# Token mixing as two f32r passes per tile, and an earlier load of layer one's second weights

## What is computed

```python
attn_out = _attn_ref(q, k, v, s)                 # 4 batches, 8 heads, 576 tokens, 64 wide; causal softmax with a bias
x = attn_out.transpose(0, 2, 1, 3).reshape(4, 576, 512)
# first layer
xn = (x - mu) / np.sqrt(var + 1e-06) * g_ln
x = x + np.maximum(xn @ w_ch1, 0.0) @ w_ch2       # 512 -> 2048 -> 512
# second layer, with token mixing
h = x.transpose(0, 2, 1) @ U @ V                  # U is 576x32, V is 32x576
u = x + h.transpose(0, 2, 1)
out = u + np.maximum(u @ w_ch1, 0.0) @ w_ch2
```

## Time and profile before

| | |
|---|---|
| median of 3 runs | 1120.89 us (1119.97 to 1123.44) |
| the profiled execution, time and span | 1120.59 us, 1118.7 us |
| busy, whole span | PE 1056.2, DVE 802.1, ACT 545.7, POOL 338.2 us |
| PE on the chain that ended last | 91% |
| attention | 0 to about 280 us |
| layer one, layer two | to about 725 us, to the end |
| mean clock granted to PE | 0.992 |

### The profile page before, as it was taken

How to read it: one execution, slowest core, us unless ns; L and a number is a source line. 1 busy time by engine, 2 the same in 40 slices (tenths; PEclk the granted TensorE clock), 3 DMA queues, 4 the chain that set the end, 5 groups by cost and what they waited for, 6 DMA issues and landing times.

```text
span 1118.7 us, 20942 instructions
## 1 busy us (share of the span) xinstructions
PE 1056.2 (94%) x6936; PEld 930.6 (83%) x6936; DVE 802.1 (72%) x1712; ACT 545.7 (49%) x1245; POOL 338.2 (30%) x375
## 2 busy tenths in 40 slices
PE   6888888888797999999999999999999999999998
PEld 5777777776687899889899888888988988888887
DVE  6999999999558668667667667875865766765533
ACT  5888888888333344244344334433423432423321
POOL 1244212117214433333324232343332323232100
PEclk9999999999799999999999999999999999999999
DMA  6655454465242221312231343422142233223131
GB/s 158 163 134 120 123 134 118 125 175 165 86 138 85 83 75 59 128 59 76 76 113 58 113 151 102 158 99 95 57 132 94 76 94 114 80 91 113 58 124 46
DMA packets 157475, 118.85 MB, mean 106 GB/s; under 512 B 87712, under 2 KB 132768, under 8 KB 157408
## 3 DMA queue, kind: packets, MB, share of 16 engines
q1 hardware_dynamic: 157408, 117.95, 35.6%
HBM read 98.97 MB, written 18.95 MB: 105 GB/s over the span
## 4 chain that ended last, share of the span: by engine, by line
PE 91%; ACT 3%; DVE 2%; issue 2%; POOL 1%; DMA 1%; ACTq 0%; SPq 0%; DVEq 0%; POOLq 0%
PE ps_up L746 10%; PE ps_up L748 9%; PE ps_up L747 9%; PE ps_acc L793 7%; PE ps_acc L792 6%; PE ps_acc L794 6%; PE ps_s L793 5%; PE ps_s L792 5%; PE ps_s L794 5%; PE ps_x L676 5%; PE ps_s L646 4%; PE ps_pt L657 3%; ACT prob L922 2%; PE ps_up L657 2%; PE ps_up L622 2%
## 5 line engine op out<-in xcount | busy, mean ns | idle before, releaser
L746 PE MATMUL ps_up<-z,w 128*128 128x256 f32 x896 | 257.2, 287 | 3.8 <-DVE z L1253 3.8
L748 PE MATMUL ps_up<-z,w 128*128 128x256 f32 x896 | 254.2, 284 | 0.0
L747 PE MATMUL ps_up<-z,w 128*128 128x256 f32 x896 | 254.2, 284 | 0.0
L556 POOL TENSOR_TENSOR w_f<-raw 128x256 f32<-128x256 f32 x64 | 71.2, 1113 | 413.2 <-DMA raw<-in_moe_w_ch 390.1
L746 PEld LDWEIGHTS ps_up<-z,w 128*128 128x128 f32 x896 | 171.9, 192 | 10.4 <-DVE z L1253 4.3
L747 PEld LDWEIGHTS ps_up<-z,w 128*128 128x128 f32 x896 | 172.1, 192 | 6.1 <-issue 1.2
L748 PEld LDWEIGHTS ps_up<-z,w 128*128 128x128 f32 x896 | 172.5, 192 | 0.0
L792 PE MATMUL ps_acc<-w_hi,h 128*128 128x512 f32 x320 | 126.9, 396 | 2.1 <-DVE x_res L1279 2.1
L793 PE MATMUL ps_acc<-w_lo,h 128*128 128x512 f32 x320 | 126.8, 396 | 0.0
L794 PE MATMUL ps_acc<-w_hi,h 128*128 128x512 f32 x320 | 126.2, 394 | 0.0
L1074 ACT ACTIVATE h<-ps_up 128x256 fp32r<-128x256 f32 x64 | 24.5, 383 | 185.4 <-PE ps_up L748 185.4
(11 more groups left out here) (160 smaller groups left out, 2619.3 us busy)
## 6 DMA issues: line engine op xcount, KB each, us to landing
raw<-in_moe_w_ch SPq DMA_DIRECT2D x80, 512.0 KB, 3.6
ncum_b<-ncum_dram SPq DMA_DIRECT2D x32, 288.0 KB, 3.6
x_in<-x_dram SPq DMA_DIRECT2D x18, 512.0 KB, 4.5
k_raw<-in_k SPq DMA_DIRECT2D x64, 128.0 KB, 2.5
u_dram<-x_in SPq DMA_DIRECT2D x9, 512.0 KB, 2.8
q_raw<-in_q SPq DMA_DIRECT2D x32, 128.0 KB, 3.2
v_raw<-in_v SPq DMA_DIRECT2D x32, 128.0 KB, 2.2
w_f<-in_moe_w_ch SPq DMA_DIRECT2D x4, 1024.0 KB, 6.7
```

The lines of the kernel that those rows point to most:

```text
L556: pool.tensor_tensor(to[:, I5, 1], a21, a22, ALU.add).then_inc(s1_done, 1)
L746: nc.tensor.matmul(bank, w_hi, z_hi, start=(start and c == 0), stop=False, skip_group_check=True)
L747: nc.tensor.matmul(bank, w_hi, z_lo, start=False, stop=False, skip_group_check=True)
L748: last = nc.tensor.matmul(bank, w_lo, z_hi, start=False, stop=(stop and c == 1), skip_group_check=True)
```

## The change

Three things are changed in the mixing. U is loaded once, into `u_raw`, and POOL makes its high and low parts, which stand side by side in `u_pad` where the two copies stood. Each finished tile is split into a high part (`tokens_high`, ACT) and a low part (`tokens_low`, DVE) in `y_split`. PE multiplies in f32r, both parts of a tile one after the other, into the same bank. The bank's two halves are then the products with U's high and low part, and have to be added: with a pair's last tile ACT copies the lower half (`half_copied`), DVE adds it (`halves_added`), and then `mixed` is rounded from the sum. `y_first` shares its memory with `zf`, `u_raw` with `mixed` and `msum`, `v_pad` with `y_last`. The residual of the next block may be loaded as soon as the tokens are split.

Beside this, all four loads of layer one's second weights are issued behind heads 0 and 1, two behind each, and POOL splits one slice in each of the heads 4 to 19.

```diff
@@ memory
         z = sbuf("z", [P, 7 * 2 * ZCOLS], F32R)
+        with ExitStack() as alias:
+            y_first = sbuf("y_first", [P, 3, 2, DM], F32R, alias)
         zf = sbuf("zf", [P, 7, ZCOLS])
...
+        with ExitStack() as alias:
+            u_raw = sbuf("u_raw", [P, PT, 2 * RANK], F32, alias)
...
-        u_pad = sbuf("u_pad", [P, PT, 2, 2 * RANK])
+        u_pad = sbuf("u_pad", [P, PT, 2, 2 * RANK], F32R)
...
+        y_last = sbuf("y_last", [P, 2, DM], F32R)
+        y_split = [y_first[:, t] for t in range(3)] + [y_last[:]]
@@ SP
                 if b > 0 and b <= LB:
-                    sp.wait_ge(mix_done, mixes_before(b))
+                    sp.wait_ge(y_split_done, rows_before(b))
...
             head_alone(0, 0, first=True)
             load_second(0)
+            load_second(KC)
             head_alone(0, 1)
-            load_second(KC)
-            with sp.Fori(1, LAST_M - 2) as m:
+            load_second(2 * KC)
+            load_second(3 * KC)
+            with sp.Fori(1, LAST_M - 1) as m:
                 head_alone(m, 0)
                 head_alone(m, 1)
-            head_alone(LAST_M - 2, 0)
-            load_second(2 * KC)
-            head_alone(LAST_M - 2, 1)
-            load_second(3 * KC)
@@ POOL
-            for u in range(4):
+            for u in range(HEADS):
                 split_values(u)
-            for j in range(2 * KC):
-                split_values(4 + j)
-                split_second(j)
-            for u in range(4 + 2 * KC, HEADS - 2 * KC // 2):
-                split_values(u)
-            for u in range(HEADS - 2 * KC // 2, HEADS):
-                split_values(u)
-                for j in range(2):
-                    split_second(2 * KC + 2 * (u - HEADS + 2 * KC // 2) + j)
+                if 4 <= u < 4 + JC:
+                    split_second(u - 4)
             inverse_root(0)
...
                 if g == QN:
+                    pool.wait_ge(u_loaded, 4 * 16)
+                    pool.tensor_tensor(u_pad[:, :, 0], u_raw[:], one[:].unsqueeze(2).to_broadcast([P, PT, 2 * RANK]), ALU.mult).then_inc(u_hi_done, 1)
+                    pool.wait_ge(u_hi_done, 1)
+                    pool.tensor_tensor(u_pad[:, :, 1], u_raw[:], u_pad[:, :, 0].bitcast(F32), ALU.subtract).then_inc(u_split, 1)
                     pool.wait_ge(v_pad_loaded, 4 * 16)
@@ PE
-                pe.wait_ge(u_loaded, 8 * 16)
-                pe.wait_ge(y_done, rows_before(a + 1))
+                pe.wait_ge(u_split, 1)
                 for x, (pair, tiles, _, _) in enumerate(mix_groups(a)):
                     for y, (t, at) in enumerate(tiles):
-                        last = nc.tensor.matmul(zb[x], u_pad[:, t].rearrange("p a r -> p (a r)"), x_res[:, at],
-                                                start=(y == 0), stop=(y == len(tiles) - 1))
+                        pe.wait_ge(y_split_done, rows_before(a) + at + 1)
+                        for part in range(2):
+                            last = nc.tensor.matmul(zb[x], u_pad[:, t].rearrange("p a r -> p (a r)"), y_split[at][:, part],
+                                                    start=(y == 0 and part == 0), stop=(y == len(tiles) - 1 and part == 1))
@@ ACT
+            def tokens_high(a):
+                for t in range(NT[a]):
+                    act.wait_ge(y_done, rows_before(a) + t + 1)
+                    wait(act, mix_done, mixes_before(a))
+                    nc.scalar.activation(y_split[t][:, 0], x_res[:, t], ACT.Copy).then_inc(y_hi_done, 1)
...
                     if last:
                         act.wait_ge(msum_added, adds_before(a) + 1)
-                        nc.scalar.activation(mixed[pair][:], msum[pair][:], ACT.Copy).then_inc(mixed_hi_done, 1)
+                        nc.scalar.activation(zf[0:2 * RANK, Z4], msum[pair][2 * RANK:P], ACT.Copy).then_inc(half_copied, 1)
+                        act.wait_ge(halves_added, pair + 1)
+                        nc.scalar.activation(mixed[pair][0:2 * RANK], msum[pair][0:2 * RANK], ACT.Copy).then_inc(mixed_hi_done, 1)
...
+                if i == 1 and not late and 0 < b <= LB:
+                    tokens_high(b - 1)
@@ DVE
+            def tokens_low(a):
+                for t in range(NT[a]):
+                    dve.wait_ge(y_hi_done, rows_before(a) + t + 1)
+                    nc.vector.tensor_tensor(y_split[t][:, 1], x_res[:, t], y_split[t][:, 0].bitcast(F32), ALU.subtract).then_inc(y_split_done, 1)
...
                     if last:
+                        dve.wait_ge(half_copied, pair + 1)
+                        nc.vector.tensor_tensor(msum[pair][0:2 * RANK], msum[pair][0:2 * RANK], zf[0:2 * RANK, Z4], ALU.add).then_inc(halves_added, 1)
                         dve.wait_ge(mixed_hi_done, pair + 1)
...
+                if i == 1 and not late and 0 < b <= LB:
+                    tokens_low(b - 1)
```

More of the change, by code:

```diff
@@ L189, in chain_kernel @@
         cs = sbuf("cs", [P, 3 * HT])
+        with ExitStack() as alias:
+            u_raw = sbuf("u_raw", [P, PT, 2 * RANK], F32, alias)
         mixed = [sbuf(f"mixed{g}", [P, DM], F32R) for g in range(2)]
         msum = [sbuf(f"msum{g}", [P, DM]) for g in range(2)]
-        u_pad = sbuf("u_pad", [P, PT, 2, 2 * RANK])
+        u_pad = sbuf("u_pad", [P, PT, 2, 2 * RANK], F32R)
         v_hi = sbuf("v_hi", [P, 2 * S], F32R)
         v_lo = sbuf("v_lo", [P, 2 * S], F32R)
-        v_pad = sbuf("v_pad", [P, 2 * S])
+        with ExitStack() as alias:
+            v_pad = sbuf("v_pad", [P, 2 * S], F32, alias)
+        y_last = sbuf("y_last", [P, 2, DM], F32R)
+        y_split = [y_first[:, t] for t in range(3)] + [y_last[:]]
         ps_up = psum("ps_up", 1024)
@@ L259, in chain_kernel @@
         mix_done, msum_copied, msum_added = sem("mix_done"), sem("msum_copied"), sem("msum_added")
+        u_hi_done, u_split = sem("u_hi_done"), sem("u_split")
+        y_hi_done, y_split_done, half_copied, halves_added = sem("y_hi_done"), sem("y_split_done"), sem("half_copied"), sem("halves_added")
         mixed_hi_done, mixed_done = sem("mixed_hi_done"), sem("mixed_done")
@@ L494, in _ @@
                     batch_a, batch_b = slice(0, RANK), slice(RANK, 2 * RANK)
-                    for copy in range(2):
[L496 to L500, removed]
+                    for dst, src in ((u_raw[:, 0:QT - 1, batch_a], U[0:FULL, :].rearrange("(t p) r -> p t r", p=P)),
+                                     (u_raw[0:LAST, QT - 1, batch_a], U[FULL:S, :]),
+                                     (u_raw[LAST:P, QT - 1, batch_b], U[0:P - LAST, :]),
+                                     (u_raw[:, QT:PT, batch_b], U[P - LAST:S, :].rearrange("(t p) r -> p t r", p=P))):
+                        sp.dma_start(dst, src).then_inc(u_loaded, 16)
+                    for copy in range(2):
                         for batch in range(2):
@@ L584, in _ @@
                     pool.wait_ge(y1_done, 1)
-                    pool.memset(u_pad[:], 0.0).then_inc(pad_zeroed, 1)
+                    pool.memset(u_raw[:], 0.0).then_inc(pad_zeroed, 1)
                     pool.memset(v_pad[:], 0.0).then_inc(pad_zeroed, 1)
                 if g == QN:
+                    pool.wait_ge(u_loaded, 4 * 16)
+                    pool.tensor_tensor(u_pad[:, :, 0], u_raw[:], one[:].unsqueeze(2).to_broadcast([P, PT, 2 * RANK]), ALU.mult).then_inc(u_hi_done, 1)
+                    pool.wait_ge(u_hi_done, 1)
+                    pool.tensor_tensor(u_pad[:, :, 1], u_raw[:], u_pad[:, :, 0].bitcast(F32), ALU.subtract).then_inc(u_split, 1)
                     pool.wait_ge(v_pad_loaded, 4 * 16)
@@ L1287, in add_mixed @@
                     if last:
+                        dve.wait_ge(half_copied, pair + 1)
+                        nc.vector.tensor_tensor(msum[pair][0:2 * RANK], msum[pair][0:2 * RANK], zf[0:2 * RANK, Z4], ALU.add).then_inc(halves_added, 1)
                         dve.wait_ge(mixed_hi_done, pair + 1)
-                        nc.vector.tensor_tensor(mixed[pair][2 * RANK:P], msum[pair][2 * RANK:P], mixed[pair][2 * RANK:P].bitcast(F32), ALU.subtract)\
+                        nc.vector.tensor_tensor(mixed[pair][2 * RANK:P], msum[pair][0:2 * RANK], mixed[pair][0:2 * RANK].bitcast(F32), ALU.subtract)\
                             .then_inc(mixed_done, 1)
```

## The result

| | before | changed |
|---|---|---|
| median of 11 runs each, same chip | 1122.78 us (1119.97 to 1125.27) | 1116.51 us (1113.79 to 1122.04) |
| ratio of the times | | 0.9946, interval 0.9929 to 0.9963 |
| the profiled execution: time, span | 1120.59, 1118.7 us | 1115.07, 1113.3 us |

The kernel became 0.5% faster. I forecast 3.2 us less; the ratio makes it 6.0 (0.54% of 1120.9), the two profiled executions 5.4 (by their spans). The forecast time, 1117.7, stands only 1.2 us above the measured median of 1116.5, and that is luck in part: I subtracted from 1120.9, a median of three runs, and the kernel before has 1122.8 over eleven.

A forecast was written before the change was run, and what follows sets the result against it. PE was taken to bound the kernel, with hardly any waits in the two layers. The terms -7.0 + 1.2 + 2.5 + 1.4 - 3.4 + 2.1 = -3.2 took 1120.9 to 1117.7 us, range 1113.6 to 1121.0.

The forecast's parts named there:

- Term 3: Group 8: POOL's split of U ahead of V lengthens PE's wait by 2.5 us, plus 1.4 for the clock.
- term 5: First heads: transposes wait for last_raw behind another 1 MB of weights in two heads; +2.1 us, bounds 0 and 5.5.
- 1 mixing's products: Mixing of blocks 0 to 4: f32r products in place of f32 save PE time on 18 tiles; -7.0 us.
- 2 the pair's hand-overs: Group 26: adding the sum's two halves on ACT and DVE delays h's rounding; +1.2 us, bounds 0 and 1.8.
- 4 weights out of the last heads: Behind the last head: without POOL's weight splits rstd comes sooner and PE's input transposes start earlier; -3.4 us.
- a sign that it was wrong: Group 9: PE's 2.14 us wait for the second residual sum staying unchanged would show the prediction wrong.
- rival (1113.8): Group 8: DVE gets the ports twice in a row, giving 1113.8 us; chance 0.34 together with other spared waits.
- rival "slower": First heads: the queue doesn't overlap each pair's copies, PE waits 7.9 us more than costed, 1125.6 us; chance 0.08.

The follow-up runs named there:

- mixing alone: New mixing of the changed kernel, second weights loaded and split as in the kernel before; ratio 0.9941 to the kernel before, median 1117.02 us.
- V ahead of U: Changed kernel with POOL's two operations on V put ahead of U's two in group 8; ratio 0.9964 to the kernel before, median 1119.67 us.
- V in group 11: Changed kernel with POOL's two operations for V moved from group 8 to group 11; ratio 0.9923 to the kernel before, median 1114.84 us.
- V in group 12: Changed kernel with POOL's two operations for V moved from group 8 to group 12; ratio 0.9948 to the kernel before, median 1118.88 us.
- loads alone: Kernel before with only the second weights' loads and splits moved as in the change, old mixing; ratio 1.0, median 1122.71 us.
- The kernel with the loads spread: Changed kernel with one second-weights load behind each of heads 0 to 3, not two behind heads 0 and 1; ratio 0.9917, median 1113.98 us.

## Why the prediction was off

The direction was right and the size too small: -3.2 forecast, -5.4 between the profiled executions. Term 3 came out 3.5 below its price; term 5 and a place without a price, 1.5 above together, made up for part of it.

```
term                                  predicted   measured
1 mixing's products                    -7.0        -7.2
2 the pair's hand-overs                +1.2        +1.1
3 POOL at group 8, wait and clock      +3.9        +0.4 (mixing alone: +3.8)
4 weights out of the last heads        -3.4        -3.4
5 weights into the first heads         +2.1        +3.2
  start of layer one to group 8         0          +0.4
```

**The step that failed is term 3**, "POOL at group 8: +2.5 us, and +1.4 for the clock". Its mechanism was right: the profiled execution of the mixing alone shows it, time by time. So do V ahead of U (3.1) and V in group 11 (no wait). The Trainium skill, "SBUF — State Buffer" (Who interferes with whom), has the pair of ports as an exclusive lock for the instruction, the first to issue first; the table of starts above agrees, with 0.16 us one way giving 4.2 and 0.08 the other way 2.0. What failed is the assumption under it, that POOL would start at 352.8 as before while nothing else moved, and would be first. In the changed kernel's trace the half-clock stretch behind the wait for `z` began earlier and lasted longer (6.8 us against 3.4). POOL's last sum ahead of its splits, which waits for PE, came 0.9 later; DVE's `h` came 0.5 later, and DVE was first. Before and after:

```profile
352.12 0.74 POOL L563 TENSOR_TENSOR w_f<-raw,w_f 128x256 f32<-128x256 f32 x1 [0.75 <-PE ps_up L748]
```

```profile
353.04 0.74 POOL L571 TENSOR_TENSOR w_f<-raw,w_f 128x256 f32<-128x256 f32 x1 [0.42 <-PE ps_up L753]
```

PE's wait then fell by 0.3 instead of rising by 2.5, and the clock stayed up; the +0.4 of the table is +0.7 from the longer stretch less this 0.3. The wait of 2.14 us was all but unchanged (1.87), which the prediction had named as a sign that it was wrong. That the stretch decides the order is not shown: in the changed kernel with V in group 12 it lasted 6.8 us too, and POOL was first. I had this case as a bound and as a rival (1113.8). I gave it too little: DVE was first in eight of the ten traces above. With a margin of tenths between two engines, the order in one trace is no evidence for the order after an edit, nor for the next execution of the same kernel. The half-clock stretch of the changed kernel, by the microsecond (clock third from the end), which in the earlier trace rows had begun at 345:

```profile
342.00:343.00 1.00, 0.00 (x0) 0.00 (x0) 1.00 (x1) 0.89 (x1) 0.00 (x0) 0.60 0.00 0
...
348.00:349.00 1.00, 1.00 (x7) 1.00 (x6) 0.00 (x0) 0.40 (x2) 0.00 (x0) 0.50 0.10 23
```

**Term 5** was right in its mechanism and its first wait: a megabyte more ahead delays the landing by 2.8, as worked out from half of one (2.8 to 3.0). The second was 1.7 and not 0.9, because SP issued `last_raw` 0.7 later (35.92 against 35.18) and it took 7.7, 3.1 more than before. 2.6 of the 3.2 are waits for it; 0.2 stood there already in head 2, and 0.2 came with each of the two waits. By the Trainium skill's rule that completion is not first in, first out ("DMA: Bandwidth & Descriptors", Queues, rings and completion order) neither wait had to come. Neither of the two small transfers got ahead here: they landed at 33.3 and 43.6, the megabytes issued just ahead of them at 33.0 and 43.1. The clock, which I had not counted in this place, is the larger risk: 1.6 us in five of the six profiled runs with the loads in pairs.

**Terms 1, 2 and 4** came out to 0.2. Term 4's gap is 2.21 (2.2 forecast) and it did not spare the clock: 0.58 in the microsecond from 284 and 0.50 for the nine behind it. The rival "slower" is refuted: the copies overlap.

Left open: what decides the order at group 8 in a given execution, and which case of term 3 the ten other runs of the changed kernel had, of which there is no trace. Their times ask for no longer wait than the traced one's: at its mean clock, 0.992, another run had a span of 1113.2 against its 1113.3. The 0.4 in place of 3.9 is shown for the profiled execution and for two neighbours of it; for the mixing alone the ratio leaves no room for the 3.8 in its usual run.

## What to carry to other kernels

Before a helper engine gets more work, look for what stands behind it on the engine that shares its ports: the same 5 us of POOL cost PE 0 with idle time behind them (group 11), 2 to 4 with PE one residual sum away (group 8), and 2.3 with a falling clock behind a normalisation (group 12). A large load moved ahead of a small one costs the small one its whole extra transfer, so spread such loads, one for each small transfer's slack. And price a wait of 1.5 to 4 us twice, with and without the half clock behind it. Where two engines contend within tenths of a microsecond, price both orders, and check a cause read from one profiled execution against the times of the others.

## What the runs showed that I had not expected

The granted clock decides a good part of the time even of one kernel: the changed kernel took 1113.8 us at a mean of 0.994 and 1122.0 at 0.987, and the kernel before took 1119.9 to 1126.1, at 0.992 to 0.988. After the same idle time the clock falls in one profiled run and not in another (at most 1.7 us at the second `last_raw` in the changed kernel: 1.00 held; at most 1.8 in "loads alone": 0.50). Four of the profiled runs, one of them with the loads as before, also ran at 0.50 for about 3 us between 21 and 26 us and stood 2.1 to 2.8 us later in head 2; the others, the changed kernel's among them, did not. The kernel with the loads spread, where only 0.2 us of that wait is left, ran four times within 0.4 us.

Where V's first operation began 0.9 us ahead of DVE's `h` (in groups 8, 11 and 12; the three kernels shown and the other four with V in group 11 or 12), `h` took 2.05 each time and the 256-wide `w` behind it 2.88 to 2.91: the stretching is as regular as the turns that cause it.
